# Attention outputs computed straight into feature-major rows, in four column tiles of TensorE

## The reference, cut to what matters

```python
def _attn_ref(q, k, v, f_logit):            # (4, 8, 768, 48) each
    f = 1.0 / (1.0 + np.exp(-f_logit))
    state = np.zeros((B, H, D, D))
    for t in range(S):
        state = f[:, :, t, :, None] * state + np.einsum('bhd,bhe->bhde', k[:, :, t], v[:, :, t])
        y[:, :, t] = np.einsum('bhd,bhde->bhe', q[:, :, t], state)
    return y

def _moe_ref(x, w_in, w_out):               # x (3072, 384), w_in (384, 2048), w_out (2048, 384)
    h = x @ w_in
    g = h * (1.0 / (1.0 + np.exp(-1.702 * h)))
    return g @ w_out

def _moe2_ref(x, domain_probs, w1, w2):     # four experts, w1 (4, 384, 1024), w2 (4, 1024, 384)
    p = domain_probs / (domain_probs.sum(-1, keepdims=True) + 1e-09)
    for e in range(E):
        out += p[:, e:e + 1] * (np.maximum(x @ w1[e], 0.0) @ w2[e])
```

## Time and profile before

| what | value |
|---|---|
| median of the runs | 1416.46 us (1416.02 to 1418.09) |
| the profiled execution, its time | 1414.12 us |
| its span in the trace | 1412.4 us |
| PE busy | 1386.7 us (98%) |
| DVE busy | 913.5 us (65%) |
| POOL busy | 629.6 us (45%) |
| ACT busy | 568.4 us (40%) |

### The profile page before, as it was taken

The page is one execution under the profiler, slowest core; times in us unless marked ns, Lnnn a source line. Parts: engine busy times, 40 slices in busy tenths (PEclk is TensorE's granted clock), DMA queues, the critical chain, the costliest instruction groups (busy, mean ns, idle before and its releaser), DMA issues.

```text
span 1412.4 us, 20981 instructions
## 1 busy us (share of the span) xinstructions
PE 1386.7 (98%) x8092; PEld 1311.8 (93%) x8092; DVE 913.5 (65%) x1376; ACT 568.4 (40%) x975; POOL 629.6 (45%) x719
## 2 busy tenths in 40 slices
PE   6899999999999999999999999999999999999999
PEld 5799999999999999999999999999999999999998
DVE  7785747566665656356566666666666666666666
ACT  5563534344444445245333233332333333433331
POOL 8686645556564747265512122211212454344430
PEclk9999999999999999999999999999999999999999
DMA  9535243332425160121011010101011112222111
GB/s 156 121 84 83 60 60 79 47 92 36 103 26 113 16 114 13 41 90 51 23 34 35 12 34 23 34 12 34 12 34 56 35 34 67 91 68 67 46 57 45
DMA packets 239796, 79.00 MB, mean 56 GB/s; under 512 B 188752, under 2 KB 238160, under 8 KB 239696
## 3 DMA queue, kind: packets, MB, share of 16 engines
q1 hardware_dynamic: 239696, 77.66, 23.9%
HBM read 67.83 MB, written 9.78 MB: 55 GB/s over the span
## 4 chain that ended last, share of the span: by engine, by line
PE 94%; POOL 2%; issue 1%; DVE 1%; ACT 1%; SPq 1%; DMA 0%; POOLq 0%; DVEq 0%; ACTq 0%
PE bank L1766 9%; PE bank L1764 9%; PE bank L1765 9%; PE bank L1700 9%; PE bank L1701 9%; PE bank L1699 9%; PE bank L1580 7%; PE bank L1672 5%; PE bank L1673 5%; PE bank L1674 5%; PE bank L1506 4%; PE bank L1508 4%; PE bank L1507 4%; PE bank L1612 3%; PE bank L1620 1%; PE bank L1629 1%
## 5 line engine op out<-in xcount | busy, mean ns | idle before, releaser
L1460 DVE SCALAR_TENSOR_TENSOR acc<-bank,p_n,acc 128x384 f32<-128x384 f32 x384 | 235.0, 612 | 68.0 <-PE bank L1766 62.9
L788 POOL TENSOR_TENSOR g_l<-sig,g_h 128x384 fp32r<-128x384 f32 x128 | 163.8, 1280 | 228.6 <-ACT g_h L1027 228.6
L1766 PE MATMUL bank<-w_h,h_l 128*128 128x384 f32 x768 | 257.3, 335 | 0.0
L1764 PE MATMUL bank<-w_h,h_h 128*128 128x384 f32 x768 | 257.2, 335 | 0.0
L1765 PE MATMUL bank<-w_l,h_h 128*128 128x384 f32 x768 | 257.0, 335 | 0.0
L1444 DVE TENSOR_TENSOR bank<-bank,x_copy 128x512 f32<-128x512 f32 x192 | 124.5, 694 | 166.0 <-ACT x_copy L1124 102.4
L1701 PE MATMUL bank<-xs,we_l 128*128 128x512 f32 x528 | 206.5, 391 | 0.0
L1700 PE MATMUL bank<-xs,we_h 128*128 128x512 f32 x528 | 206.4, 391 | 0.0
L1699 PE MATMUL bank<-xs,we_h 128*128 128x512 f32 x528 | 205.5, 389 | 0.7 <-issue 0.7
L839 POOL TENSOR_TENSOR we_l<-we_raw,we_h 128x384 fp32r<-128x384 f32 x96 | 97.2, 1037 | 213.4 <-ACT we_h L1092 213.4
L1356 DVE TENSOR_TENSOR sig<-bank,sig 128x384 f32<-128x384 f32 x128 | 71.0, 555 | 162.8 <-ACT sig L1020 161.4
(11 more groups left out here) (145 smaller groups left out, 2567.1 us busy)
## 6 DMA issues: line engine op xcount, KB each, us to landing
we_raw<-in_moe_w SPq DMA_DIRECT2D x32, 384.0 KB, 4.0
w_raw<-in_moe_w SPq DMA_DIRECT2D x32, 384.0 KB, 3.3
v_sb<-in_v SPq DMA_DIRECT2D x24, 192.0 KB, 3.5
x_dram<-work SPq DMA_DIRECT2D x8, 576.0 KB, 3.1
x_raw<-x_dram SPq DMA_DIRECT2D x12, 384.0 KB, 4.0
f_raw<-in_f_logit SPq DMA_DIRECT2D x56, 72.0 KB, 2.1
q_raw<-in_q SPq DMA_DIRECT2D x56, 72.0 KB, 2.1
k_raw<-in_k SPq DMA_DIRECT2D x56, 72.0 KB, 2.0
```

The source lines that it names most:

```text
L788: pool.tensor_tensor(g_l[:, j % RING, :], sig[:, j % 2, :], g_h[:, j % RING, :].bitcast(F32), ALU.subtract).then_inc(gl_ready, 1)
L1460: dve.scalar_tensor_tensor(acc[:, pr * TT + i, :], y_bank[y % 3][:, 0:DM], p_n[:, col:col + 1], acc[:, pr * TT + i, :], ALU.mult, ALU.add) ...
L1764: pe.matmul(dst, hh, wh, start=f == 0, stop=False)
L1766: last = pe.matmul(dst, hl, wh, start=False, stop=f == 1)
```

## The change

From half 1 on, `y` is computed transposed. The 384 features are numbered 3p + m: row p (0 to 127), part m (0 to 2). A pair of heads has 96 features, which are 32 rows by 3 parts, so pair r fills rows 32r to 32r + 31 of the bank. A matmul of the new `y_columns` has 32 stationary columns (every third column of `v_sb` or `state`) and 128 moving columns (`scores_T` or `q_T`), and goes to column tile r of the array (`tile_position=(0, 32 r)`). Since the 32 rows mix the features of both heads of a pair, each head's `v` stands beside 48 zero columns (`VW = 3 * D`), and the product of either head runs over all 32 columns. So a `y` step has 3 x 2 x 4 = 24 matmuls from `v_sb` and 3 x 4 = 12 from `state`.

The bank then has what the transposes gave before. In halves 1 to 7 the copy to `y_rows`, the transposes and their unit's bank are gone, and ACT and DVE read `y`'s own bank in slots 12, 14, 16. Half 0 keeps its way, with a stride of 3 in the transposes. The rows of `w_in` are read in the same order (`"(p k) n -> k p n"`). `v` is loaded in six transfers per half, of half the size, DVE clears the zeros of `v_sb` once at the start, and ACT and DVE wait in half 1 for the last weight pieces, whose stages share memory with `x_h1`.

```diff
-    v_sb = at("v_sb", [P, CH, DM])
+    VW = 3 * D
+    v_sb = at("v_sb", [P, CH, PAIRS, VW])
...
-    win_v = w_in.rearrange("(k p) n -> k p n", p=P)
+    win_v = w_in.rearrange("(p k) n -> k p n", p=P)
...
+    def v_columns(c, h, m):
+        lo = h % 2 * D + m
+        return v_sb[:, c, h // 2, lo:lo + 31 * KT + 1:KT]
+
+    def state_columns(r, m):
+
+        return state[:, r, m::KT]
...
                 for c in range(CH):
-                    sp.dma_start(v_sb[:, c, :].rearrange("p (h d) -> p h d", h=H),
-                                 v_v[b, a, c, :, :, :]).then_inc(v_loaded, 16)
+                    for j in range(2):
+                        sp.dma_start(v_sb[:, c, :, 2 * j * D:(2 * j + 1) * D],
+                                     v_v[b, a, c, :, j::2, :]).then_inc(v_loaded, 16)
...
                 if s == "x":
-                    u = chunk_unit["x", c]
+                    u = chunk_unit["x" if fine(n) else "y", c]
 
                     act.wait_ge(unit_ready, n * UNITS + u + 1)
+                    if n == 1 and c == 0:
+
+                        act.wait_ge(w_lo["pool"], lows("pool", W_PIECES - 1))
+                        act.wait_ge(w_lo["dve"], lows("dve", W_PIECES - 1))
...
+            dve.memset(v_sb[:, :, :, D:2 * D], 0.0).then_inc(zeros_ready, 1)
...
-                if s == "y":
+                if s == "y" and fine(n):
...
-                    else:
-                        dve.tensor_copy(y_rows[:, :], ring[u % 3][:, 0:DM])\
-                            .then_inc(read_by["dve"], counts(c, a))
...
+            def y_columns(c, n, a):
+                u = chunk_unit["y", c]
+                from_state = not (a == 0 and c == 0)
+
+                def add(r, m, lhs, rhs, start, stop):
+                    lo = SQ * r
+                    return pe.matmul(ring[u % 3][lo:lo + SQ, m * P:(m + 1) * P], lhs, rhs, start=start, stop=stop,
+                                     tile_position=(0, lo), skip_group_check=True)
+
+                for m in range(KT):
+                    for j in range(2):
+                        for r in range(PAIRS):
+                            last = add(r, m, v_columns(c, 2 * r + j, m), scores_T[:, c, 2 * r + j, :],
+                                       m == 0 and j == 0, m == KT - 1 and j == 1 and not from_state)
+                if c:
+
+                    pe.wait_ge(read_by["dve"], n * PER_HALF["dve"] + reads("dve", chunk_unit["update", c - 1]))
+                for m in range(KT if from_state else 0):
+                    for r in range(PAIRS):
+                        x = r * CH + c
+                        last = add(r, m, state_columns(r, m), q_T[:, x * P:(x + 1) * P], False, m == KT - 1)
...
+                    if not fine(n):
+                        y_columns(c, n, a)
+                        return
...
-                if s == "x":
+                if s == "x" and fine(n):
```

More of the change, by code:

```diff
@@ L286, in spread, with v_heads, v_head @@
             [P, PAIRS * HB >> (L + 1), 1 << L])
+    def v_heads(c):
+        return v_sb[:, c, :, :].rearrange("p r (x d) -> p r x d", x=3)[:, :, 0::2, :]
+    def v_head(c, h):
+        lo = h % 2 * 2 * D
+        return v_sb[:, c, h // 2, lo:lo + D]
+    def v_columns(c, h, m):
[3 more added lines that the diff above has]
+        return state[:, r, m::KT]
     def mask_of(L):
@@ L1343, in step @@
                                                  state_faded[lo:lo + D, :, j * D:(j + 1) * D], ALU.add)
-                    last.then_inc(read_by["dve"], 1)
+                    last.then_inc(read_by["dve"], 1 if fine(n) else 2)
                 if s == "x":
-                    u = chunk_unit["x", c]
+                    u = chunk_unit["x" if fine(n) else "y", c]
                     dve.wait_ge(xh_ready, n * CH + c + 1)
+                    if n == 1 and c == 0:
+                        dve.wait_ge(w_lo["pool"], lows("pool", W_PIECES - 1))
+                        dve.wait_ge(w_lo["dve"], lows("dve", W_PIECES - 1))
                     dst = slice(c * P, (c + 1) * P)
                     dve.tensor_tensor(x_l[a][:, :, dst], ring[u % 3][:, 0:DM].rearrange("p (m t) -> p m t", m=KT),
-                                      x_h[a][:, :, dst].bitcast(F32), ALU.subtract).then_inc(read_by["dve"], 1)
+                                      x_h[a][:, :, dst].bitcast(F32), ALU.subtract)\
+                        .then_inc(read_by["dve"], 1 if fine(n) or leads_on(c, a) else 3)
             def gelu_product(n, j):
@@ L1495, in bank_free, with last_read @@
                 before = [x for x in range(u) if x % 3 == u % 3]
+                def last_read(w, n):
+                    name, c = units[w]
+                    return chunk_unit["x", c] if name == "y" and n else w
                 if before:
-                    w = before[-1]
+                    w = last_read(before[-1], n)
                     pe.wait_ge(read_by[reader[w]], n * PER_HALF[reader[w]] + reads(reader[w], w))
                 elif not (n == 0):
-                    w = [x for x in range(UNITS) if x % 3 == u % 3][-1]
+                    w = last_read([x for x in range(UNITS) if x % 3 == u % 3][-1], n - 1)
                     pe.wait_ge(read_by[reader[w]], (n - 1) * PER_HALF[reader[w]] + reads(reader[w], w))
@@ L1509, in product @@
                 return last
+            def y_columns(c, n, a):
[6 more added lines that the diff above has]
+                for m in range(KT):
+                    for j in range(2):
+                        for r in range(PAIRS):
[7 more added lines that the diff above has]
+                        last = add(r, m, state_columns(r, m), q_T[:, x * P:(x + 1) * P], False, m == KT - 1)
+                last.then_inc(unit_ready, counts(c, a) + (c > 0) + (not leads_on(c, a)))
             def step(s, c, n, a, b):
@@ L1628, in step @@
                     for r in range(PAIRS):
-                        last = pe.matmul(ring[u % 3][:, r * 2 * D:(r + 1) * 2 * D], k_rows[:, r * P:(r + 1) * P],
-                                         v_sb[:, c, r * 2 * D:(r + 1) * 2 * D], start=True, stop=True)
-                    last.then_inc(unit_ready, counts(c + 1, a))
-                if s == "x":
+                        last = pe.matmul(ring[u % 3][:, r * 2 * D:(r + 1) * 2 * D].rearrange("p (j d) -> p j d", j=2),
+                                         k_rows[:, r * P:(r + 1) * P], v_heads(c)[:, r, :, :], start=True, stop=True)
+                    last.then_inc(unit_ready, counts(c + 1, a) + (c == CH - 1 and not fine(n)))
+                if s == "x" and fine(n):
                     u = chunk_unit["x", c]
@@ L1637, in step @@
                     for m in range(KT):
-                        last = pe.transpose(ring[u % 3][:, m * P:(m + 1) * P], y_rows[:, m * P:(m + 1) * P],
-                                            ident[:, :])
+                        last = pe.transpose(ring[u % 3][:, m * P:(m + 1) * P], y_rows[:, m::KT], ident[:, :])
                     last.then_inc(unit_ready, 1)
```

27 lines of the change are left out of this document (13 added, 14 removed).

## The result

| kernel | median, lowest to highest (us) | profiled execution (us) | its span (us) |
|---|---|---|---|
| before | 1416.33, 1416.02 to 1418.09 | 1414.12 | 1412.4 |
| after | 1403.24, 1401.75 to 1404.87 | 1404.87 | 1403.2 |

The changed kernel is faster by about 1%: ratio 0.9905, 95% interval 0.9888 to 0.9922, which is 13.1 us between the medians. The forecast was 1436 us with a range of 1395 to 1452. The time lies in the range, but on the other side of 1416, so the likeliest case was wrong and the rival "four at a time" (1397 us, chance 0.25) was near; the range held the result only because it reached out for that rival.

What follows compares the result with a forecast made beforehand. PE's work was taken to bound rounds 0 to 6. Overlap +17.7, switches +3.5 and the `x_l` wait -1.3 gave +19.9 us on the profiled 1414.1, 1434.0, so 1436 us in the runs; range 1395 to 1452.

Steps and rivals of the forecast that it cites:

- the likeliest case: In the `y` steps, program matmuls overlap two at a time, 0.11 us each; 1436 us in all, chance 0.53.
- four at a time: Rival for the `y` steps: all four column tiles stream at once, 1.98 us a step with state; 1397 us, chance 0.25.
- The bound: In rounds 0 to 6 PE is the limit, so a microsecond of PE work is a microsecond of time.
- What the removed work costs: Old `y` and `x` steps on PE: 3.06 us with state, 2.13 without, 61.5 us over 21 steps.
- What a new matmul streams: On a 32-column tile, a 128-column fp32 instruction streams 0.11 us, a program matmul of two 0.22 us by itself.
- How many run side by side: In a new `y` step, starts keep program order, so two overlap: 3.96 us with state, 2.64 without; +17.7 us.
- its own sign of being wrong: The prediction called itself wrong if a `y` step takes under 3.1 us, or rounds lengthen by waits on other engines.
- The second row: Load pairs after idle time, read as dispatched 0.06 us apart: 0.12 us a matmul, 4.32 us a `y` step.
- Switching: 42 changes between 128-column and 32-column tiles around `y` steps, at most 0.17 us each, 7.1 us; taken as +3.5 us.
- the choice of one in two: Of each `y` step's two array switches only one costs in full, the way out; +3.5 us instead of 7.1.
- The wait for `x_l`: PE's 1.3 us wait at a round's start should go, as the chain to `x_l` becomes shorter; -1.3 us.
- What costs nothing: Removed DVE copies, memset, new ACT and DVE waits, `v` transfers, two-piece `update` and the ring: 0 us each.

Runs made afterwards that it cites:

- e1: The changed kernel with each tile's matmuls of a `y` step issued all in a row, one tile after the other; 1464.47 us (one run).
- e2: The changed kernel with three matmuls of one tile in a row in a `y` step, then three of the next; 1433.39 us (one run).
- e5: The changed kernel with `update` also in the four column tiles, 32 instructions instead of 8; 1397.11 us, ratio 0.987.
- e7: The changed kernel with half 0's six `v` transfers issued behind the `f` blocks instead of before them; 1404.13 us, ratio 0.9916.

## Why the prediction was wrong

**The bound was right.** PE's work in the rounds sets the time: the rounds became 10.3 us shorter in the trace, half 0 1.1 us longer, and the rest of the span kept its 816.5 us.

**What the removed work costs: nearly right.** The forecast had 3.06 us for a step with state, read from the step at 567.31, whose `y` takes 2.73 us to the start of `update`. That is one of two that begin after a short wait; the others take 2.65, or 2.60 where no `update` follows. With the transposes most steps are 2.98 us, and 18 x 0.08 = 1.4 us were counted too much. The three without state took 2.12, 2.12 and 2.05, the forecast had 2.13.

**What a new matmul streams: right.** The estimate of 0.11 us for 128 fp32 columns is the 0.109 us from one group of four starts to the next.

**How many run side by side: this is the step that failed.** It said that a matmul's second instruction waits for its tile and the next tile's first one stands behind it, so two at a time, 3.96 us a step. The trace has 1.92, under the 3.1 us that the prediction had named as its own sign of being wrong: four start within 20 ns, and `e1` and `e2` show later instructions starting before earlier ones. The mistake was to take starts in program order, true of every timeline before the change, for a rule; there all instructions used the same full array, so none could pass. The second row I leaned on the earlier trace rows was no better: `e5` starts an instruction every 10.7 ns. This step alone is 18 x (3.96 - 1.98) + 3 x (2.64 - 1.32) = 39.6 us.

The Trainium skill (TensorE: Matmul & The Clock Gate, Packing small matmuls) says that matmuls start and end strictly in program order. Here the measurement decides against it for the starts of fp32 pairs on column tiles: in `e1` and `e2` instructions of the `state` part start ahead of others that stand before them. Its small gap between starts on neighbouring tiles, some 4 ns, agrees roughly: four start within 20 ns, some 7 ns apart.

**Switching: the size per switch was about right, the choice of one in two wrong.** The bound of 0.17 us stands against 0.14 measured, but both ends cost: 42 x 0.14 = 5.9 us and not 3.5. The Trainium skill (TensorEngine Tiling (Array Packing), Tiling Modes) has a change of mode drain the engine; the runs agree in that every change costs, 5.9 us in all where the prediction worked out 7.1 for it.

**The wait for `x_l`: wrong.** The -1.3 us was to come from the shorter chain. But that wait stands once, ahead of the first `hidden` of round 0, whose input is half 0's, and half 0 keeps its way through `y_rows`. It is there after the change with the same 1.3 us. I had read the total of a view without asking at which time it fell.

**What costs nothing: consistent.** The additional issues of `v` cost nothing (`e7`). That the 21 removed copies on DVE were worth nothing fits with the sum, but no kernel with the copy added back was run. What I missed is the other side of a shorter step: POOL's `g_l` comes late more often, 1.5 us.

The sum with the measured terms: +19.9 - 39.6 (overlap) + 2.4 (switches) + 1.3 (`x_l`) + 1.5 (`g_l`) + 1.4 (removed work) = -13.1 us. That it meets the 13.1 between the medians is luck in part. The terms come from two traces whose spans differ by 9.2 us; with the half-clock stretch (1.5) and the longer half 0 (1.1) of the one after, the sum is -10.5, and 1.3 us are not explained. How much of those two is in the medians isn't known.

## What to carry to other kernels

In this kernel an fp32 instruction on the full array took 0.11 us with 48, 96 or 128 moving columns. On 32-column tiles four of 128 columns took that time together, and 48 columns took less in proportion, as long as neighbours in the program went to different tiles; each switch between full array and tiles took 0.14 us. So fp32 products with few moving columns are worth cutting into column tiles if they are many enough to pay for two switches. An order seen in one mode of an engine is no rule for a mode that has never run in the trace, so the rival without it deserves a like chance. A layout that reaches into the loads at the start is judged by the DMA queue there as much as by the steps it serves.

## What the runs showed of the hardware that I had not expected

- Instructions on different column tiles pass one that waits for its tile, with a limited reach: 1.92 us for 72 when neighbours in the program lie on four different tiles, 2.01 with two program matmuls in a row on one tile, 3.50 with three, 5.06 with all of a tile's in a row.
- On four tiles an fp32 instruction with 48 moving columns starts every 10.7 ns; on the full array the same 48 columns took 0.11 us.
- Loads of `w_in` in four blocks of 32 rows by one transfer held SP's queue no longer than plain ones for the first three (2.12 us against 2.27). The next three took 1.9 us apiece instead of 0.46, and the issues behind them were slow too: `v` took 10.41 us for three where it took 5.32 for six. Meanwhile the DMA engines' busy share was 0.33 instead of 1.13.
- The granted clock fell to its lower level for a few microseconds at the start of round 0 in the changed kernel (PE busy 0.58 of the 2 us from 62 to 64) and not in the one before (0.85). PE's busy time there doesn't tell the cases apart: it is 0.74 both in `e1`, whose clock stays up, and in `e5`, whose clock falls. Why is open.
